# Folded weights kept whole in DRAM and split at the second network's beginning

## The reference

```
attn = softmax over a window of 56 keys and 8 memory keys, chunk of 32 queries   # 4 x 8 heads, 768 tokens, 64 wide
x    = attn, as 3072 tokens x 512
# first network: w_in 512 x 2048, w_out 2048 x 512
h = x @ w_in
g = (a0 + a1 h + a2 h^2 + a3 h^3) / (1 + |b0| |h| + |b1| h^2 + 1e-6)
x = g @ w_out
# second network: w1, w2 512 x 1024, w3 1024 x 1024, w_out2 1024 x 512
out = ((x @ w1) * (x @ w2)) @ w3 @ w_out2
```

## Time and profile before

| | |
|---|---|
| median of 3 runs | 1122.7 us (1122.17 to 1123.64) |
| the profiled execution | 1123.65 us, its span 1121.9 us |
| PE busy | 1088.7 us (97%) |
| DVE busy | 706.8 us (63%) |
| ACT busy | 583.1 us (52%) |
| POOL busy | 169.0 us (15%) |
| mean granted TensorE clock | 0.988 |

### The profile page before, as it was taken

The page is one execution under the profiler, slowest core; times in us unless marked ns, Lnnn a source line. Parts: engine busy times, 40 slices in busy tenths (PEclk is TensorE's granted clock), DMA queues, the critical chain, the costliest instruction groups (busy, mean ns, idle before and its releaser), DMA issues.

```text
span 1121.9 us, 16471 instructions
## 1 busy us (share of the span) xinstructions
PE 1088.7 (97%) x6292; PEld 896.0 (80%) x6292; DVE 706.8 (63%) x995; ACT 583.1 (52%) x960; POOL 169.0 (15%) x137
## 2 busy tenths in 40 slices
PE   8999987899999999999999999999999999999998
PEld 6877766687888888888888888888888888888886
DVE  5378875899999999999998998811212121111211
ACT  3457763677876876877787787521213122121311
POOL 4324542412122122121100100100000000000000
PEclk9999996899999999999999999999999999999999
DMA  9989994211211220121100146320202010020000
GB/s 308 265 210 248 275 259 123 75 57 48 84 56 47 71 69 28 56 85 46 56 37 0 37 150 221 116 76 1 75 0 75 0 37 37 0 75 0 37 1 38
DMA packets 138733, 97.65 MB, mean 87 GB/s; under 512 B 89548, under 2 KB 118220, under 8 KB 137676
## 3 DMA queue, kind: packets, MB, share of 16 engines
q1 hardware_dynamic: 126028, 90.92, 26.8%
q10 hardware_dynamic: 12672, 6.29, 1.9%
HBM read 65.74 MB, written 31.46 MB: 87 GB/s over the span
## 4 chain that ended last, share of the span: by engine, by line
PE 51%; DVE 25%; issue 4%; ACT 2%; ACTq 0%; DVEq 0%
PE banks L1199 23%; PE banks L1214 11%; PE banks L1183 9%; PE banks L205 8%; DVE nr L1102 5%; DVE nr L1099 5%; DVE nr L1106 4%; DVE g_lo L1111 3%; DVE sq L1082 3%; DVE poly L1089 3%; DVE poly L1092 1%; DVE x_lo L1068 1%; ACT y_sb L1004 1%; ACT habs L978 0%; ACT sq L981 0%
## 5 line engine op out<-in xcount | busy, mean ns | idle before, releaser
L1183 PE MATMUL banks<-g_hi,weights 128*128 128x512 f32 x768 | 253.4, 392 | 4.9 <-DVE g_lo L1111 4.8
L205 PE MATMUL banks<-x_hi,weights 128*128 128x512 f32 x768 | 253.6, 393 | 1.9 <-PEq L215 1.9
L1199 PE MATMUL banks<-x_hi,weights 128*128 128x512 f32 x768 | 244.2, 389 | 0.0
L1140 DVE TENSOR_TENSOR nr<-habs,banks 128x512 f32<-128x512 f32 x48 | 33.0, 688 | 256.7 <-ACT habs L1034 256.7
L1183 PEld LDWEIGHTS banks<-g_hi,weights 128*128 128x128 f32 x768 | 144.9, 189 | 37.7 <-DVE g_lo L1111 7.2
L205 PEld LDWEIGHTS banks<-x_hi,weights 128*128 128x128 f32 x768 | 145.7, 190 | 32.5 <-issue 2.0
L1199 PEld LDWEIGHTS banks<-x_hi,weights 128*128 128x128 f32 x768 | 144.1, 188 | 29.8
L1034 ACT ACTIVATE habs<-banks 128x512 f32<-128x512 f32 x48 | 28.6, 596 | 245.2 <-PE banks L1199 245.2
L205 PE MATMUL banks<-x_lo,weights 128*128 128x512 f32 x384 | 150.6, 392 | 0.0
L1183 PE MATMUL banks<-g_lo,weights 128*128 128x512 f32 x384 | 150.0, 391 | 0.0
L1199 PE MATMUL banks<-x_lo,weights 128*128 128x512 f32 x384 | 149.4, 389 | 0.0
(11 more groups left out here) (83 smaller groups left out, 1544.0 us busy)
## 6 DMA issues: line engine op xcount, KB each, us to landing
x_raw<-x_transposed_dram SPq DMA_DIRECT2D x12, 1024.0 KB, 5.3
weights<-second_mlp_weights_dram SPq DMA_DIRECT2D x8, 1536.0 KB, 6.3
second_mlp_weights_dram<-split SPq DMA_DIRECT2D x16, 512.0 KB, 3.0
v_sb<-in_v SPq DMA_DIRECT2D x44, 160.0 KB
qk_sb<-in_q SPq DMA_DIRECT2D x24, 256.0 KB, 4.7
x_transposed_dram<-xt_sb ACTq DMA_DIRECT2D x24, 256.0 KB, 4.2
x_transposed_dram<-y_sb SPq DMA_DIRECT2D x6, 1024.0 KB, 4.9
out<-y_sb SPq DMA_DIRECT2D x5, 1024.0 KB, 4.2
```

What stands on the lines that cost most here:

```text
L205: last = nc.tensor.matmul(bank[m % 4][:, :], slot[:, m, a, cols], x[:, c, :], start=c == 0 and n == 0, stop=c == KC - 1 and n == 2)
L1183: last = nc.tensor.matmul(bank[4 + c][:, :], slot[:, m, a, cols], g[:, m % G_BUFS, :], start=m == 0 and n == 0, stop=m == SLOTS - 1 and n ...
L1199: last = nc.tensor.matmul(bank[2 * (j % 2) + w][:, :], bslot[:, j, 2 + 2 * w + a, cols], x[:, c, :], start=c == 0 and n == 0, stop=c == KC ...
```

## The change

The fold stores the folded weights as one float32 tensor, 256 KB for each i, 2 MB in all. VectorE's subtraction in the fold is gone. At the handover SP loads for each slot the four tiles of w1 and w2 into place (1024 KB) and the whole folded weights (256 KB) into one of three buffers, `wf_raw` (`stage` in the code), which take the place of GpSimd's `raw` and `split`. ScalarE makes hi (`wf_hi`), VectorE lo (`wf_lo`), four slots before slot 0's work and four after it. `finish_c` waits for `wf_lo_ready`.

```diff
+WF_BUFS = 3
...
-        wf = fold("wf", [P, 2, 2, DM], F32R)
+        wf = fold("wf", [P, 2, DM])
...
             def store_wf(i):
-                sp.wait_ge(wf_split, i + 1)
-                sp.dma_start(bweights[i, :, 0:2 * BLK], f32(wf[:, i % 2, :, :].rearrange("p a b -> p (a b)")))\
-                    .then_inc(wf_stored[i % 2], 16)
+                sp.wait_ge(wf_copied, i + 1)
+                sp.dma_start(bweights[i, :, 0:BLK], wf[:, i % 2, :]).then_inc(wf_stored[i % 2], 16)
...
-            def wf_hi(i):
+            def copy_wf(i):
                 act.wait_ge(folded, i + 1)
                 act.wait_ge(wf_stored[i % 2], i // 2 * 16 + 16)
-                nc.scalar.activation(wf[:, i % 2, 0, :], bank[4 + i % 2][:, :], ACT.Copy).then_inc(wf_hi_ready, 1)
+                nc.scalar.activation(wf[:, i % 2, :], bank[4 + i % 2][:, :], ACT.Copy).then_inc(wf_copied, 1)
...
-            def wf_lo(i):
-                dve.wait_ge(wf_hi_ready, i + 1)
-                nc.vector.tensor_tensor(out=wf[:, i % 2, 1, :], in0=bank[4 + i % 2][:, :],
-                                        in1=f32(wf[:, i % 2, 0, :]), op=ALU.subtract).then_inc(wf_split, 1)
...
-            pe.wait_ge(wf_split, JS)
+            pe.wait_ge(wf_copied, JS)
...
+        stage = Place(nc, pl.at, pl.end)("wf_raw", [P, WF_BUFS, BLK])
...
                 last_slot = ((j + 1) * BSLOT - 1) // (4 * BLK)
                 sp.wait_ge(w_out_done, (NBLK - 1) * (SLOTS - 1) + last_slot + 1)
-                sp.dma_start(f32(bslot[:, j, :, :]), bweights[j, :, :].rearrange("p (a c) -> p a c", a=6))\
+                sp.dma_start(f32(bslot[:, j, 2:6, :]), bweights[j, :, 2 * BLK:].rearrange("p (a c) -> p a c", a=4))\
                     .then_inc(slot_loaded[j], 16)
+                if j >= WF_BUFS:
+                    sp.wait_ge(wf_lo_ready, j - WF_BUFS + 1)
+                sp.dma_start(stage[:, j % WF_BUFS, :], bweights[j, :, 0:BLK]).then_inc(wf_loaded[j % WF_BUFS], 16)
...
+            def wf_hi(j):
+                act.wait_ge(wf_loaded[j % WF_BUFS], j // WF_BUFS * 16 + 16)
+                act.wait_ge(slot_loaded[j], 16)
+                nc.scalar.activation(bslot[:, j, 0, :], stage[:, j % WF_BUFS, :], ACT.Copy).then_inc(wf_hi_ready, 1)
+
+            for j in range(4):
+                wf_hi(j)
             copy_a(0, 0)
             copy_y(NBLK - 1)
             c_his(0, 0)
+            for j in range(4, JS):
+                wf_hi(j)
             step_b(0, 0)
...
+            def wf_lo(j):
+                dve.wait_ge(wf_hi_ready, j + 1)
+                nc.vector.tensor_tensor(out=bslot[:, j, 1, :], in0=stage[:, j % WF_BUFS, :], in1=f32(bslot[:, j, 0, :]),
+                                        op=ALU.subtract).then_inc(wf_lo_ready, 1)
+
+            for j in range(4):
+                wf_lo(j)
             make_c(0, 0)
+            for j in range(4, JS):
+                wf_lo(j)
             step_b(0, 0)
...
             def finish_c(i, j):
                 pe.wait_ge(c_lo_ready, i * JS + j + 1)
+                pe.wait_ge(wf_lo_ready, j + 1)
```

More of the change, by code:

```diff
@@ L264, in attention_and_weights @@
         w3_hi_ready, w3_split = sem("w3_hi_ready"), sem("w3_split")
-        folded, wf_hi_ready, wf_split = sem("folded"), sem("wf_hi_ready"), sem("wf_split")
+        folded, wf_copied = sem("folded"), sem("wf_copied")
         q_loaded, k_loaded, memk_loaded = sem2("q_loaded"), sem2("k_loaded"), sem("memk_loaded")
@@ L523, in _ @@
                     copy_turned(0, n // TURNED, n % TURNED)
-                wf_hi(i)
+                copy_wf(i)
             exp(0, 1)
@@ L651, in _ @@
                     tile_step(0, 0)
-                wf_lo(i)
             def coefficients():
@@ L782, in _ @@
                 if i > 1:
-                    pe.wait_ge(wf_split, i - 1)
+                    pe.wait_ge(wf_copied, i - 1)
                 pe.wait_ge(w3_split, i * 2 + 2)
@@ L842, in mlps @@
         raw_loaded, raw_hi_ready, raw_split = sem("raw_loaded"), sem("raw_hi_ready"), sem("raw_split")
+        wf_loaded = [sem(f"wf_loaded{u}") for u in range(WF_BUFS)]
+        wf_hi_ready, wf_lo_ready = sem("wf_hi_ready"), sem("wf_lo_ready")
         split_stored, ones_ready = sem("split_stored"), sem("ones_ready")
```

## The result

| | before | changed |
|---|---|---|
| median | 1123.17 us (1122.17 to 1123.74, 4 runs) | 1129.22 us (1126.85 to 1130.21, 4 runs) |
| ratio of the times | | 1.0053, 95% interval 1.0037 to 1.0068 |
| the profiled execution | 1123.65, span 1121.9 | 1126.85, span 1124.7 |
| mean granted TensorE clock | 0.988 | 0.991 |
| PE busy | 1088.7 us | 1086.0 us |

The change made the kernel slower by 4.2 to 7.6 us. A second set of runs gave 1127.91 against 1120.63 us, 1.0067 [1.0054, 1.0079] (experiment 5).

What follows compares the result with a forecast made beforehand. TensorE was taken to bound the kernel, so whatever stops it is paid in full. Fold 0, handover stall 2.8 and low clock 1.7 were added: 1122.7 + 0 + 2.8 + 1.7 = 1127.2 us, range 1123.4 to 1129.6.

Steps and rivals of the forecast that it cites:

- The clock: Behind the stall at the handover: TensorE's granted clock falls to 0.5 for some 3.4 us, 1.7 us lost.
- The fold: In the fold: removing VectorE's eight subtractions and halving eight stores saves 0; at one end 0.5 us lost.
- The sign that failed: At the first network's end: forecast is wrong if it comes over 1 us earlier or later than before.
- SP's waits: On SP at the handover: small load 3 goes out at 728.1 us, small load 7 at 737.05.
- The first gate: Before `finish_c(0,0)`: `c_lo` ends at 736.35, TensorE asks at 736.70; 0.35 us left, no stall.
- The queue: Loads at the handover: 5.51 MB at 399 GB/s take 13.8 us, plus 2.4 fixed; last landing at 744.3 us.
- The stall: Before `finish_c(0,1)`: `c_lo` ends at 747.6, TensorE asks at 744.86; one stall of 2.8 us.
- stall without the clock: Rival at the handover: the 2.8 us stall comes but no low clock, 1125.5 us; chance 0.17.
- The queue is faster: Rival at the handover: quicker queue or small loads passing large ones, landing by 741.5, no stall, 1122.7 to 1124.0; chance 0.16.
- 265 GB/s case: Slow-queue end at the handover: stall 9.8 us, time 1134.2; shares chance 0.10 with 360 GB/s, mostly the latter.
- The queue is slower: Rival at the handover: 360 GB/s gives stall 4.3, 1128.7 us; 265 gives 9.8, 1134.2; chance 0.10 in all.
- Faster: Rival in the attention: earlier v loads remove two TensorE waits and low clocks, 8.6 us gained, 1118.6; chance 0.04.

Runs made afterwards that it cites:

- experiment 5: The changed kernel run again with nothing altered, beside the kernel before: 1127.91 us against 1120.63, 1.0067 [1.0054, 1.0079].
- Experiment 3: Changed kernel without staging buffers: whole folded weights loaded in place with the other four tiles, one transfer per slot, same splits; 1120.99 us against 1121.3, 0.9999.
- experiment 1: Changed fold with the handover's early loads as before, two transfers per slot, no splits, lo part left out of the product; 1122.3 us against 1121.3, 1.001.
- Experiment 4: Changed kernel with SP's large loads 4 to 7 issued ahead of the small loads that wait; 1121.09 us, 1.0006 [0.9993, 1.0018].
- experiment 2: Fold of the kernel before, both parts stored, with the changed handover splitting hi again; 1128.45 us against 1121.3, 1.0068 [1.0049, 1.0087].
- experiment 9: Kernel before with 24 extra copies on ScalarE ahead of slot 1's copy of a; idle gap 2.69 us, ratio 1.002 [1.0001, 1.0039].
- 20 and 22 extra copies: Kernel before with that many added copies on ScalarE ahead of slot 1's copy of a; ratios 1.0021 and 1.0027.
- 24, 25 and 26: Kernel before with that many added copies on ScalarE ahead of slot 1's copy of a; ratios 1.002, 1.0043 and 1.0058.
- experiment 11: In-place loading version of the change, with GpSimd's splits held back until the attention's second tile is normalised; 1122.21 us against 1121.72, 1.0009.
- experiment 12: Kernel before with 25 extra copies on ScalarE ahead of slot 1's copy of a; idle gap 3.21 us, ratio 1.0043 [1.0026, 1.006].

## Why the prediction was right, and where not

The mechanism holds: small loads that wait, all transfers behind them, copies ahead of slot 1's copy of a, one stall at `finish_c(0,1)`. The time lies within the stated range, near its upper end; the 7.3 us of the second set would be just past it (1129.6 less 1122.7 is 6.9). That the low clock came on top is in part luck, as shown under *The clock*.

Times in this part count from the start of the last `g_hi` (726.06 before and in the prediction, 723.88 in the changed kernel).

- **The fold, 0.** It holds within 1 us. Experiment 3, with the new fold and no stall, gives 0.9999 [0.9989, 1.0009]; experiment 1 leaves room for up to 2 us, experiment 3 for 1.0. TensorE's transposes behind the check start at 70.73 us, 70.91 in the earlier trace rows, and again it is a copy of k that they wait for. One reading of the program was wrong without harm: the check after the last fold is not the only place where TensorE waits for the subtraction. `pe.wait_ge(wf_split, i - 1)` stands before each fold from i = 2 on, but in the trace of before TensorE never waited there.
- **The sign that failed.** The prediction calls itself wrong if the first network ends over 1 us earlier or later than before, and in the profiled execution it ended 2.2 us earlier. The sign was chosen too narrow: identical instructions differ by up to 5.4 us at this place (table above), and the means of both folds differ by 0.1.
- **SP's waits.** Small load 3 was to go out at 2.04 us and went at 1.99, small load 7 at 10.99 and went at 10.04.
- **The first gate.** `wf_hi(3)` was to start at 5.54 and did at 5.10; `c_lo` of slot 0 was to end 0.35 us before TensorE asks and ended 1.2 us before. The four y copies, no longer held up by a bank, took 2.05 us in one go, not 2.29. No stall, as said.
- **The queue, 16.2 us to the last landing.** This step was sized short: 16.75 us (725.87 to 742.62). The last landing came at 18.74, not 18.24, although its load had gone out 1 us sooner. The windows show 385 and 418 GB/s where I took 399, then 311. I had counted 5.5 MB of loads and left out the store of x2, 1 MB, which I had myself named as standing behind these waits: it goes out at 734.29, only 0.4 us behind small load 7, and shares the queue with it. Until 739 us the queue kept the rate of the earlier trace rows; from there to the last landing it moved 217 and then 341 GB/s. Experiment 4 gives a hint of what the store costs a load just ahead of it: with the large loads gone, the five waiting small loads landed after a median of 3.0 us, and the last of them, with the store 0.4 us behind it, after 3.6 (734.70 to 738.32). That is the 0.6 us by which this step was short, but a kernel without the store was not run.
- **The stall, 2.8 us.** Measured 3.4 us, and 3.7 idle in experiment 2. The chain from the copy to `c_lo` took 3.34 us, 3.3 as worked out; the error lies in the queue's step.
- **The clock, 1.7 us.** The number is right (1.6 and 1.7 us behind the two gaps of 3.2 us), its reason is not. I expected the low clock behind a stall of 2.8 us, since it had followed on idle gaps of 1.80 and 1.93 us in the attention and between the stages. In this dense stretch 2.69 us is forgiven, and 3.20 us is not. Had the stall been as short as I worked it out (2.8 us, of which some 2.6 would show as idle), the rival *stall without the clock* would have come by experiment 9. Two errors met: a stall sized 0.6 us too short, and gaps from less dense stretches taken as the measure for this one.
- **The sum.** 4.5 us forecast, 5.0 in the profiled section, 6.0 by the medians (1129.22 less 1123.17). Of the rest, 0.3 us lies outside the span: mean of time less span is 2.07 us in the changed kernel's runs and 2.04 to 2.13 in all versions that load a slot by two transfers, but 1.76 to 1.80 in before and all others, the one in place among them. The remainder, 0.7 us here and about 1.4 in experiment 5 (mean span 1125.78 against 1119.13, 6.65 us, of which the section shows 5.2), stays open. Experiment 2, with the old fold, has 1.3 (6.9 against 5.6). It can't be put down to the handover's transfers: 20 and 22 extra copies, with none of them, leave 1.0 and 1.3 (1.9 and 3.2 against 0.9 and 1.9), while 24, 25 and 26 leave -0.5, -0.2 and 0.1. So it is of the size by which medians and single traces differ here.
- **The rivals.** *The queue is faster* did not come, nor the 265 GB/s case. *The queue is slower* was half right, by some 0.5 us. *Faster* did not come. In the attention (70 to 199 us) these are TensorE's two groups with the longest waits, before:

```profile
L753 PE MATMUL banks<-pT,v_sb 96*64 96x64 f32 x768 | 29.3, 233 | 6.7 <-DMA v_sb<-in_mem_v 5.2 <-ACT pT L495 1.5
L740 PE MATMUL banks<-ident,probs 128*96 128x128 f32 x192 | 28.2, 295 | 3.9 <-DVE probs L626 3.9
```

and changed:

```profile
L747 PE MATMUL banks<-pT,v_sb 96*64 96x64 f32 x768 | 28.9, 231 | 5.0 <-ACT pT L495 3.6 <-DMA v_sb<-in_v 1.4
L734 PE MATMUL banks<-ident,probs 128*96 128x128 f32 x192 | 27.2, 287 | 8.2 <-DVE probs L621 8.1
```

The wait for v loads did shrink, as that rival asks, from 5.2 to 1.4 us, but the wait for VectorE's probabilities grew from 3.9 to 8.1. None of it can be put down to the change, since the shares go to and fro with either fold. With the change's, experiment 11 has 4.8 us of `in_mem_v` again and 4.5 of VectorE, and with the old one experiment 12 has no wait for v at all and 12.6 us of VectorE:

```profile
L753 PE MATMUL banks<-pT,v_sb 96*64 96x64 f32 x768 | 28.5, 229 | 1.6 <-ACT pT L495 1.6
L740 PE MATMUL banks<-ident,probs 128*96 128x128 f32 x192 | 28.2, 295 | 12.7 <-DVE probs L626 12.6
```

The Trainium skill's page "TensorE: Matmul & The Clock Gate", section HAM oscillation — how this bites in real kernels, warns of idle gaps longer than any of those that were forgiven here (0.61, 1.65 and 2.69 us), and so far the traces agree with it. The gaps of 3.20, 3.21 and 3.35 us, which brought the low clock, are a little shorter than the page says, and there the measurement decides. I had weighed the attention's gaps against the page; for this dense stretch it was the better guide.

## What to carry to other kernels

A staged buffer that is reused turns a load that was early into one that waits for a consumer, and on an in-order issuing engine it also delays every transfer behind it: first list what stands behind the wait, and put what needs no wait ahead (experiment 4), or let the load land where nothing has to come free (experiment 3). When a stall is worked out, add up all transfers that share the queue until the last landing, stores included. In a dense stretch of matmuls the last half microsecond of a stall can cost four times its length: here 2.69 us idle cost 3.0, and 3.21 cost 5.1. And before a shift of some microseconds in one trace is explained, look how far traces of identical programs lie apart at that place.

## What the runs showed of the hardware that was not expected

- The granted clock stayed at 1.00 behind idle gaps of 0.61, 1.65 and 2.69 us in a dense stream of 512-wide matmuls, and was 0.50 (the lower level, 1.2 GHz) behind gaps of 3.20, 3.21, 3.35, 3.70 and 3.73 us. It lasted 3.3 to 3.5 us behind the first four, and 6.1 behind 3.73 us. Behind 3.20, 3.21 and 3.73 us it was there (0.50 to 0.55) from the first matmuls on; behind 3.35 and 3.70 us TensorE first ran at the full clock again (means of 0.85 and 0.79 over the first 1.4 and 1.7 us). In the attention and between the stages, where the matmuls are not as dense, it followed on gaps of 1.80 and 1.93 us. Each of these lengths was traced once, so whether the same gap always ends the same way is not shown.
- A load of 256 KB took 3.1 us where little stood ahead of it in the queue (725.87 to 728.98), about as in the earlier trace rows, and 8.7 us behind the large ones (733.92 to 742.62): the small load did not pass them.
- Versions whose slots are loaded by two transfers each took 0.3 us more outside the span than those with one. Why is not known.
